# First chunk of a three-layer kernel: another order of block products, first writes by ScalarE, first operands split tile by tile

## The reference

```
attn   = causal 7-tap convolution of x along the sequence, taps = softmax(weight) per head
theta  = attn @ w_theta                       # 192 x 192
zr, zi = attn * cos(theta), attn * sin(theta)
y      = w_tok_r @ zr + w_tok_i @ zi          # along the sequence, nearly all of the work
u      = attn + y;   x2 = u + relu(u @ w_ch)
u2     = x2 + low-rank mixing of x2 (rank 32)
out    = u2 + relu(u2 @ w_ch1) @ w_ch2
```

## Time and profile before

| what | value |
|---|---|
| time of three runs | median 2811.42 us (2810.92 to 2813.18) |
| the profiled execution's own time | 2811.03 us |
| its span in the profile | 2809.2 us |
| mean granted TensorE clock over the span | 0.991 of full |
| busy: PE, DVE, ACT, POOL | 2748.8, 2173.6, 1015.4, 217.7 us |
| share of the chain that ended last: PE, DVE, issue, DMA, ACT | 91%, 5%, 2%, 1%, 1% |

### The profile page before, as it was taken

One profiled execution on the slowest core, in us unless ns is written; L12 is line 12 of the kernel. 1 busy time (PEld: TensorE's weight loads), 2 busy tenths in 40 slices (PEclk: granted clock), 3 DMA queues, 4 the chain that ended last, 5 costly groups with the idle time before them and its releaser, 6 DMA issues.

```text
span 2809.2 us, 37144 instructions
## 1 busy us (share of the span) xinstructions
PE 2748.8 (98%) x14533; PEld 2651.4 (94%) x14533; DVE 2173.6 (77%) x2481; ACT 1015.4 (36%) x1373; POOL 217.7 (8%) x252
## 2 busy tenths in 40 slices
PE   6999999999999999999999999999999999999999
PEld 4889999999999999999999999999999989999999
DVE  7878878878888789788788887986767875666665
ACT  4333333333333333333333333333232443333433
POOL 4000101001101001010010010010100000000000
PEclk8999999999999999999999999999999999999999
DMA  6656757768668677677686686775862000100000
GB/s 176 171 141 181 182 162 188 177 171 219 152 185 191 151 196 179 168 189 172 175 211 155 187 188 166 192 168 167 198 163 76 34 3 20 38 27 29 27 29 34
DMA packets 102351, 396.10 MB, mean 141 GB/s; under 512 B 10657, under 2 KB 28737, under 8 KB 102081
## 3 DMA queue, kind: packets, MB, share of 16 engines
q0 software_dynamic: 31680, 143.29, 29.5%
q1 hardware_dynamic: 70528, 250.83, 25.2%
HBM read 355.15 MB, written 38.93 MB: 140 GB/s over the span
## 4 chain that ended last, share of the span: by engine, by line
PE 91%; DVE 5%; issue 2%; DMA 1%; ACT 1%; SPq 0%; DVEq 0%; ACTq 0%
PE bank L1135 22%; PE bank L1136 22%; PE bank L1134 22%; PE bank L1226 2%; PE bank L1229 2%; PE bank L1230 2%; PE bank L1228 2%; PE bank L1227 2%; PE bank L1086 2%; PE bank L1211 1%; PE bank L1214 1%; PE bank L1213 1%; PE bank L1215 1%; PE bank L1212 1%; DMA w_raw<-in_w_tok 1%
## 5 line engine op out<-in xcount | busy, mean ns | idle before, releaser
L1134 PE MATMUL bank<-w_h,z_op 128*128 128x424 f32 (+1 forms) x3465 | 1234.2, 356 | 9.2 <-DVE z_op L812 4.7
L1135 PE MATMUL bank<-w_l,z_op 128*128 128x424 f32 (+1 forms) x3465 | 1230.9, 355 | 0.0
L1136 PE MATMUL bank<-w_h,z_op 128*128 128x424 f32 (+1 forms) x3465 | 1230.1, 355 | 0.0
L510 ACT ACTIVATE w_h<-w_raw 128x1272 fp32r<-128x1272 f32 x385 | 487.4, 1266 | 1151.3 <-PE bank L1136 1037.3
L1134 PEld LDWEIGHTS bank<-w_h,z_op 128*128 128x128 f32 x3465 | 652.5, 188 | 28.1 <-issue 5.7
L1135 PEld LDWEIGHTS bank<-w_l,z_op 128*128 128x128 f32 x3465 | 652.3, 188 | 17.2
L1136 PEld LDWEIGHTS bank<-w_h,z_op 128*128 128x128 f32 x3465 | 652.0, 188 | 15.9
L817 DVE TENSOR_TENSOR w_l<-w_raw,w_h 128x1272 fp32r<-128x1272 f32 x385 | 569.0, 1478 | 57.5 <-ACT w_h L510 57.4
L480 POOL DMA_DIRECT2D w_raw<-in_w_tok x220 | 193.4, 930 | 1899.6 <-DVE w_l L817 1344.4
L847 DVE TENSOR_TENSOR Y<-Y,bank 128x1272 f32<-128x1272 f32 (+1 forms) x110 | 162.0, 1473 | 134.2 <-PE bank L1136 129.1
L1018 DVE SCALAR_TENSOR_TENSOR hid_l<-bank,hid_h 128x384 fp32r<-128x384 f32 x264 | 144.4, 557 | 149.6 <-ACT hid_h L694 146.3
(11 more groups left out here) (120 smaller groups left out, 2987.0 us busy)
## 6 DMA issues: line engine op xcount, KB each, us to landing
w_raw<-in_w_tok SPq DMA_DIRECT2D x220, 636.0 KB, 4.3
w_raw<-in_w_tok POOLq DMA_DIRECT2D x220, 636.0 KB, 6.4
z_raw<-z_out SPq DMA_DIRECT2D x85, 576.0 KB, 6.7
z_out<-zf SPq DMA_DIRECT2D x66, 384.0 KB, 6.4
x_win<-in_xin SPq DMA_DIRECT2D x22, 585.0 KB, 5.7
out<-res SPq DMA_DIRECT2D x22, 576.0 KB, 2.8
v_raw<-in_v SPq DMA_DIRECT2D x11, 144.0 KB, 2.6
w_raw<-in_w SPq DMA_DIRECT2D x1, 1536.0 KB, 6.8
```

The lines of the kernel that those rows point to most:

```text
L510: nc.scalar.activation(w_h[:, s % WRING], w_raw[:, SLOT[s]], ACT.Copy).then_inc(wh_ready, 1)
L1134: mm(o, zh, wh, start=(k == 0 and not goes_on), stop=False, skip_group_check=goes_on)
L1135: mm(o, zh, wl, start=False, stop=False, skip_group_check=goes_on)
L1136: last = mm(o, zl, wh, start=False, stop=(k == KC - 1), skip_group_check=goes_on)
```

## The change

Chunk 0 gets an order of its own. Its first ten stages are products 5 and 6, which need only the plain blocks and the three units of one group; the group of pair 0 is now group 0. The units of group 1 are computed within the loop, at stages 4, 6 and 8. Group 0's convolution is two tiles on DVE and one on PE, group 1's is one on PE before the loop and two on DVE at stages 0 to 2. The z operands of the first three products are split unit by unit (`piece_hi`, `piece_lo`), and PE waits for each piece on its own.

The memsets are gone. What first writes an accumulator is a copy on ACT from PSUM (`touch`), for products 0, 4, 5 and 6 of chunk 0; DVE then has one addition less for each of them. For product 0 the touch waits for DVE's remaining addition, and it stands ahead of `w_hi(s + 2)` in ACT's list. PE waits for both before it writes those banks again.

The due stages of chunk 0's and chunk 1's preparations move. Group 4's and 5's units are now due on PE at s = 38, 41, 44 and 52, 55, 58; their products stay three stages behind, at 41, 44, 47 and 55, 58, 61. An instruction that loads ACT's table for the sine is placed before the first w_hi. From stage 70 on nothing is moved.

```diff
-STAGES = [(c, q, g) for c in range(CHUNKS) for q, g in STEPS]
+FIRST_STEPS = [(5, 0), (5, 1), (6, 0), (6, 1), (5, 2), (5, 3), (6, 2), (6, 3), (5, 4), (6, 4), (0, 0), (0, 1), (0, 2),
+               (0, 3), (1, 0), (1, 1), (1, 2), (1, 3), (2, 0), (2, 1), (2, 2), (2, 3), (0, 4), (3, 0), (1, 4), (4, 0),
+               (2, 4), (3, 1), (3, 2), (4, 1), (4, 2), (3, 3), (3, 4), (4, 3), (4, 4)]
+ALONE = (0, 6, TG - 1)
+STAGES = [(0, q, g) for q, g in FIRST_STEPS] + [(c, q, g) for c in range(1, CHUNKS) for q, g in STEPS]
...
+    sums, touches = (2 if q == 0 else 1), 0
+    if c == 0 and q in (0, 4, 5, 6) and (c, q, g) != ALONE:
+        sums, touches = sums - 1, (2 if (q, g) == (5, TG - 1) else 1)
+    EVACS.append((EVACS[-1] if EVACS else 0) + sums)
+    TOUCHES.append((TOUCHES[-1] if TOUCHES else 0) + touches)
...
+OPERANDS = ((5, 6, 0, 1, 2, 3, 4), tuple(range(PRODUCTS)))
+PIECED = 3
+def operand(c, q):
+    return PRODUCTS * c + OPERANDS[min(c, 1)].index(q)
+def splits_done(o):
+    return KC * (o + 1) if o < PIECED else KC * PIECED + o - PIECED + 1
...
+def conv_tiles(n):
+    return {0: (0, 1), 1: (1, 2)}.get(n, (0, 1, 2))
...
-    if n == 3:
-        return 17 + k // 2
-    return {2: 1, 4: 28, 5: 43}.get(n, PER * (n // 2 - 1) - 11 + 17 * (n % 2)) + k
+    if n in (1, 2, 3):
+        return {1: (0, 0, 1, 1, 2, 2, 2), 2: (10, 11, 12, 13, 13, 14, 15), 3: (20, 21, 22, 23, 24, 25, 26)}[n][k]
+    return {4: 31, 5: 45}.get(n, PER * (n // 2 - 1) - 11 + 17 * (n % 2)) + k
...
+EARLY = 4
 def theta_stage(n, r):
-    if n in (2, 3, 4, 5):
-        return {2: 8, 3: 21, 4: 35, 5: 50}[n] + (3 if n == 3 else 4) * r
+    if n < 6:
+        return {1: (4, 6, 8), 2: (16, 18, 20), 3: (27, 29, 31), 4: (38, 41, 44), 5: (52, 55, 58)}[n][r]
     return conv_stage(n, 0) + (8, 13, 17)[r]
 def angle_stage(n, r):
-    return theta_stage(n, r) + 1
+    return theta_stage(n, r) + (0 if n < EARLY else 1)
 def product_stage(n, r):
-    return theta_stage(n, r) + (2 if n == 3 else 3)
+    return theta_stage(n, r) + (1 if n < EARLY else 3)
...
 def group_pair(n):
-    return 1 - n % 2
+    return n if n < 2 else 1 - n % 2
...
+                if n == 2:
+                    sp.wait_ge(conv_ready, 1)
...
+                elif n >= 3:
+                    sp.wait_ge(conv_ready, 2)
+                    sp.wait_ge(sin_step, 6)
...
+            sp.dma_start(theta_w[:], w_theta).then_inc(const_loaded, 16)
+            load_w(0)
+            load_w(1)
             load_x(1)
-            sp.dma_start(theta_w[:], w_theta).then_inc(const_loaded, 16)
-            for n in range(RAWS):
-                load_w(n)
-            for m in range(KC):
-                store_z(m // KC, m % KC)
-            load_z(0, 3)
+            load_w(2)
+            store_z(0, 0)
+            load_w(3)
+            load_w(4)
+            store_z(0, 1)
+            store_z(0, 2)
             load_x(2)
...
-            for s in range(3):
-                sum_w(s)
-            pool.wait_ge(conv_tap, TP)
-            for j in range(TILES):
-                for a in range(0, SEQ, SEQ // 4):
-                    nc.gpsimd.memset(Y[:, j, a:a + SEQ // 4], 0.0).then_inc(zeroed, 1)
-            for s in range(3, NS):
+            for s in range(NS):
...
+            def touch(s):
+                _, q, g = STAGES[s]
+                n, lo, hi = width(g), g * TW, HALF + g * TW
+                c11, c21 = Y[:, 0:TP, lo:lo + n], Y[:, 0:TP, hi:hi + n]
+                to = {5: c21, 6: c11, 0: Y[:, TP:, lo:lo + n], 4: Y[:, TP:, hi:hi + n]}[q]
+                sums = psum[:, TP * (s % 2):TP * (s % 2) + TP, 0:n]
+                act.wait_ge(acc_ready, s + 1)
+                if q == 0:
+                    act.wait_ge(acc_free, EVACS[s])
+                if (q, g) == (5, TG - 1):
+                    nc.scalar.activation(c11, sums, ACT.Copy).then_inc(touched, 1)
+                nc.scalar.activation(to, sums, ACT.Copy, scale=-1.0 if q in (0, 5) else 1.0).then_inc(touched, 1)
...
+            def piece_hi(o, r):
+                if o < 2:
+                    act.wait_ge(product, 2 * r + (2 if o == 0 else 1))
+                    src = zf_of(r)[:, o]
+                else:
+                    act.wait_ge(z_added, r + 1)
+                    act.wait_ge(conv_tap, conv_done(1))
+                    act.wait_ge(product, 4)
+                    src = z_raw[:, 0, r]
+                nc.scalar.activation(z_op[o][:, 0, r], src, ACT.Copy).then_inc(zh_ready, 1)
...
+            for n, t in enumerate((2, 0)):
                 for k in range(TAPS):
-                    nc.scalar.activation(diag[:, TAPS * t + k], ident[:], ACT.Copy,
+                    nc.scalar.activation(diag[:, TAPS * n + k], ident[:], ACT.Copy,
                                          scale=tap[:, t, k:k + 1]).then_inc(diag_ready, 1)
+            nc.scalar.activation(sines[:, 0, 0:1], tap[:, 0, 0:1], ACT.Sin).then_inc(table_ready, 1)
             w_hi(0)
             copy_conv(0)
+            turn(0)
+            turn(1)
+            sin(0)
+            turn(2)
+            piece_hi(0, 0)
+            copy_conv(1)
+            sin(1)
+            piece_hi(0, 1)
+            sin(2)
+            piece_hi(0, 2)
             w_hi(1)
-            turn(0)
-            copy_conv(1)
-            sin(0)
-            turn(1)
-            sin(1)
-            turn(2)
-            copy_conv(2)
-            sin(2)
-            z_hi(0, 0)
-            turn(3)
-            sin(3)
-            turn(4)
-            sin(4)
+            for r in range(KC):
+                piece_hi(1, r)
...
+                if s >= 1 and TOUCHES[s - 1] > (TOUCHES[s - 2] if s > 1 else 0):
+                    touch(s - 1)
+                for n in range(1, EARLY):
+                    for r in range(KC):
+                        if product_stage(n, r) == s:
+                            sin(KC * n + r)
                 if s + 2 < NS:
                     w_hi(s + 2)
...
+                if c == 0:
+                    dve.wait_ge(touched, TOUCHES[_stage[0, 0 if q == 2 else 5, g]])
+                if s == PER:
+                    dve.wait_ge(touched, TOUCHES[-1])
+                if s and EVACS[s - 1]:
                     dve.wait_ge(acc_free, EVACS[s - 1])
...
                     vec.tensor_tensor(c21, c21, sums, ALU.subtract).then_inc(acc_free, 1)
-                    vec.tensor_tensor(h, h, sums, ALU.subtract).then_inc(acc_free, 1)
+                    if c:
+                        vec.tensor_tensor(h, h, sums, ALU.subtract).then_inc(acc_free, 1)
...
             w_lo(0)
             angles(0)
-            w_lo(1)
             angles(1)
             products(0)
-            first_sum(0)
+            piece_lo(0, 0)
             angles(2)
             products(1)
-            first_sum(1)
+            piece_lo(0, 1)
             products(2)
-            first_sum(2)
-            angles(3)
-            z_lo(0, 0)
-            products(3)
-            first_sum(3)
-            angles(4)
-            add_residual(0, 0)
-            products(4)
-            first_sum(4)
+            piece_lo(0, 2)
+            w_lo(1)
+            for r in range(KC):
+                piece_lo(1, r)
...
                     for n in range(GP):
-                        if s == (1 if n == 0 else 3 if n == 1 else residual_stage(n) + 1):
+                        if s == residual_stage(n) + 1:
                             dve.wait_ge(residual, SUMS_BEFORE[n + 1])
-                    evacuate(s - 1)
+                    if EVACS[s - 1] > (EVACS[s - 2] if s > 1 else 0):
+                        evacuate(s - 1)
+                for n in range(2):
+                    if residual_stage(n) == s:
+                        add_residual(n, s)
+                for n in range(1, EARLY):
+                    for r in range(KC):
+                        if product_stage(n, r) == s:
+                            products(KC * n + r)
+                            if n == 1:
+                                first_sum(KC * n + r)
                 if s + 2 < NS:
                     w_lo(s + 2)
...
-                        if product_stage(n, r) == s:
+                        if n >= EARLY and product_stage(n, r) == s:
                             products(KC * n + r)
...
+                angle_bank, x = theta_bank(m), x_bank(m)
+                pe.wait_ge(conv_tap, conv_done(n))
                 if n == 1:
-                    pe.wait_ge(attn_ready, TP)
-                else:
-                    pe.wait_ge(conv_tap, conv_done(n))
-                if m == 2:
+                    pe.wait_ge(attn_ready, 2)
+                if m >= KC:
+                    pe.wait_ge(product, 2 * m)
+                mm(angle_bank, src[:, 1, rows], theta_w[:, D:3 * D], start=True, stop=False)
+                mm(angle_bank[:, 0:D], src[:, 0, rows], theta_w[:, 0:D], start=False, stop=False)
+                if n == 0:
                     pe.wait_ge(attn_ready, 1)
...
-            conv_1(0)
-            conv_1(1)
+            conv_pe(0)
```

(100 more changed lines are left out.)

201 lines of the change are left out of this document (91 added, 110 removed).

## The result

| | before | after |
|---|---|---|
| median of 17 runs each, us | 2811.64 | 2816.54 |
| lowest and highest | 2809.38 to 2813.18 | 2814.59 to 2817.85 |
| span of the profiled execution | 2809.2 | 2815.7 |

The ratio is 1.0019, with a 95% interval of 1.0012 to 1.0025: slower by 3 to 7 us. The forecast was 2816.

What follows compares the result with a forecast made beforehand. PE was taken to bound the kernel apart from its first 470 us. Start -30.9, stages 1 to 34 +4.6 and chunk 1 +31.2 gave +4.9 us on 2811.0, plus 0.4 for the median: 2816 us, range 2803 to 2828.

Steps and rivals of the forecast that it cites:

- -30.9 + 4.6 + 31.2 = +4.9: Forecast changes in us against the kernel before: the start, stages 1 to 34, chunk 1, and their sum.
- The step by step list: Before stage 1: instruction times worked through for ACT, PE and DVE, putting stage 1 at 32.4 us against 63.26.
- 2.5 us of lower clock: Stages 0 to 2: PE gaps in stage 0 make some run at the lower clock; booked in stages 1 to 34.
- forecast 12.1: Stages 13 to 16: PE waits 12.1 us in all because DVE falls behind, standing still 2.4 us at touches.
- the one at 27: Stage 27: the same count of DVE's work for s = 21 to 26 leaves PE a wait of 1.7 us.
- clock 6 x 2.0 = 12.0: Chunk 1: six PE waits each cost 2.0 us of lower clock, 12.0 us in all.
- wait of over 2 us: PE: any idle wait this long also lowers the clock afterwards, priced at 2.0 us a wait.
- 191.4 and 193.4: Undisturbed PE time in us: stages 1 to 34 with nine units, and chunk 1 with seven units.
- The first (the clock holds): Faster: no clock drop at the new waits, giving back 16.5 us, 2799.8 us; chance 0.16.
- The second (touches of 0.5): No change: touches take 0.5 us and the 1.7 at s = 27 goes, 4.5 us less, 2811.8; chance 0.12.
- The third (lower clock twice as long): Slower: lower clock lasts twice as long at each wait, 6 x 2.0 us more, 2828 us; chance 0.13.
- The fourth (the clamp has another cause): Slower: the clamp's wait is not the memsets' and stays, start 10.2 us later, 2826.5 us; chance 0.06.

Runs made afterwards that it cites:

- e5: Changed kernel with 12 of the 24 memsets put back on POOL in an unbroken row; 2820.7 us in one run.
- e9: Kernel before, with each of its 24 memsets on POOL waiting for the one before it; 2803.5 us.
- e2: Changed kernel with w_hi(s + 2) ahead of the touch in ACT's list behind stages of product 0; 2805.8 us.
- e7: Changed kernel with the first write of product 0's second accumulator moved from ACT back to DVE; 2812.3 us.
- e1: Changed kernel with products of groups 4 and 5 due two stages behind their unit instead of three; 2790.2 us.
- e4: Changed kernel with the edits of e1 and e2, and units of groups 4 and 5 due on PE one stage later; 2776.3 us.
- e8: e4 with chunk 1's second z operand loaded, summed and split one stage earlier and its fourth split one stage later; 2776.0 us.

## Why the prediction was right

**The sum.** Forecast -30.9 + 4.6 + 31.2 = +4.9; measured -29.7 + 3.1 + 32.5 = +5.9 at stage 70, 4.9 between the medians.

**The start.** The step by step list held. Its 2.5 us of lower clock were booked behind stage 1; 1.7 fell into stage 0, and so stage 1 came 1.1 us late. The share of the clamp is shown by e5 and e9 (8.4 us at stage 0 in the kernel before). Of the rest of the 29.7 us (plain weight block, three units, pieces) no run takes one part alone.

**Stages 1 to 34.** DVE standing still for 2.4 us behind product 0 was 2.51 in a row, the touch taken at 1.2 was 1.24. PE's waits at stages 13 to 16 were 1.36 + 2.79 + 1.55 + 4.33 = 10.0 of a forecast 12.1; the one at 27 was 1.76 of 1.7, small waits 0.3 of 1.0. The clock behind the waits of 2.79 (0.82 from 110.57 to 120.0) and 4.33 (0.67 from 128.93 to 138.0) lost 1.7 + 3.0 = 4.7 us, where 4.5 stood in the sum. So the waits were 2.8 us too long in it, the clock 0.2 too short, and 1.1 us of the 209.25 has no term. e2 and e7, which take the cause away in two ways, show that it was the cause.

**Chunk 1.** Waits, forecast and measured: 4.2 and 3.95 (s = 38), 4.1 and 3.99 (41), 5.4 and 5.25 (44), 3.0 and 2.74 (52), 4.1 and 4.23 (55), 4.1 and 3.99 (58); 24.9 and 24.15. e1 removes the four that come from due stages; e4 takes the one at 52 away and, with e8, only moves the one at 38. The term "clock 6 x 2.0 = 12.0" measured 13.0: the five stretches shown under e1, 10.3, and 2.7 behind stage 38 (0.74 from 262.6 to 273.0). The stretch's mean of 0.93 alone would say 16.2, but it also counts low clock while PE stood idle, which costs nothing more. 193.4 + 24.15 + 13.0 = 230.6 of 231.6; 1.0 us has no term here either.

**What the prediction misread.** The price is not one number. Its "wait of over 2 us" cost 1.7 to 3.0 us of clock in the changed kernel, 1.7 behind 2.18 us in e4, and nothing behind 2.36 in e4 and 2.72 in e1. The 0.72 and 1.59 us that it calls steps are lengths of records: the steps at the lower clock are 0.35. And after the 4.68 us of before not most of two stages ran slow but 13 of the 27 matmuls of one, to 83.3 us. With the rounded terms that are printed, its 191.4 and 193.4 come out as 191.2 and 193.2.

**The rivals.** The first (the clock holds) fell with the clock behind all six waits of chunk 1. The second (touches of 0.5) fell with 1.24; its price too was doubtful, as the wait at s = 27 stayed when e2 took the touches of product 0 out of DVE's way. The third (lower clock twice as long) fell with 13.0 instead of 24 us. The fourth (the clamp has another cause) fell with the clamps of 0.36 us after the change, and e5 showed the cause.

The forecast was nearly right for a change made of three large terms that cancel: -30, +3, +32. The mechanisms were the ones that it named. That the sum came out within 1 us is partly luck, as waits 3.6 us too long met a clock 2.9 us too little, 2.1 us that no term held, and pieces at the start that were about 0.6 us early. The fastest versions are e4 and e8, 2776.3 and 2776.0 us, 1.2% below before.

## What to carry to other kernels

When an operation moves to an idler engine, look at what stands behind it in that engine's list and who waits for that; a write of 1.2 us cost the busy engine 2.5 until it was put one place later. When due stages are tightened, check that a consumer at step s never needs what a producer does at the same s behind the evacuation of the step just ended: each such place cost PE a wait of 4 to 5 us and about 2 us of clock. Gains at the start of a long loop are only kept if the stretch behind it is counted as well.

## What was not expected of the hardware

A row of 12 memsets on POOL held one DVE clamp of 128 x 384 for 6.18 us, until the row was over; with the same 12, each waiting on a semaphore for the one before, a clamp took 0.72 to 1.08 us, at a price of 1.6 us for the row (12.66 against 11.04). The clamp is a one-input operation from SBUF to SBUF; the two-input instructions around it, from PSUM or SBUF, kept their 0.56 us during the memsets.
